# Splitting half of an expert's first w2 earlier, and longer filler runs of TensorE at the start, in an attention and two-MoE kernel

## The reference

```python
# attention in blocks of 64 tokens, 4 batches, 8 heads, 576 tokens, 64 features
scores = scale * np.matmul(q_c, k_c.transpose(0, 1, 2, 4, 3))
attn = softmax(scores); out = np.matmul(attn, v_c)
# x: 2304 tokens x 512 features
a = x @ w_a; b = x @ w_b          # 512 x 1536 each
x = a * b @ w_out                 # 1536 x 512
p = domain_probs / (domain_probs.sum(-1, keepdims=True) + 1e-09)
for e in range(4):                # w1[e]: 512 x 1024, w2[e]: 1024 x 512
    h = np.maximum(x @ w1[e], 0.0)
    out += p[:, e:e + 1] * (h @ w2[e])
```

## Time and profile before

| | us |
|---|---|
| median of 3 runs | 1179.96 |
| lowest, highest | 1179.81, 1180.49 |
| profiled execution, its own time | 1181.31 |
| span of its trace, first to last instruction | 1179.5 |
| TensorE busy in it | 1168.0 |
| VectorE, ScalarE busy | 858.8, 502.5 |
| mean granted TensorE clock | 0.998 of full speed |

### The profile page before, as it was taken

How to read it: one execution, slowest core, us unless ns; L and a number is a source line. 1 busy time by engine, 2 the same in 40 slices (tenths; PEclk the granted TensorE clock), 3 DMA queues, 4 the chain that set the end, 5 groups by cost and what they waited for, 6 DMA issues and landing times.

```text
span 1179.5 us, 18721 instructions
## 1 busy us (share of the span) xinstructions
PE 1168.0 (99%) x7577; PEld 1127.7 (96%) x7577; DVE 858.8 (73%) x1147; ACT 502.5 (43%) x869; POOL 0.7 (0%) x6
## 2 busy tenths in 40 slices
PE   8999999999999999999999999999999999999998
PEld 7999998889999889999999999999999999999997
DVE  5786789888788893367877777797346677777787
ACT  6555464445534542244444434444233533333332
POOL 0000000000000000000000000000000000000000
PEclk9999999999999999999999999999999999999999
DMA  7396785879877699938777777648894877676761
GB/s 270 118 348 239 284 321 222 327 301 348 339 300 271 260 412 362 331 131 324 307 262 251 279 279 274 241 166 285 254 356 170 340 264 263 251 266 250 262 252 55
DMA packets 73162, 319.54 MB, mean 271 GB/s; under 512 B 7340, under 2 KB 13812, under 8 KB 56692
## 3 DMA queue, kind: packets, MB, share of 16 engines
q1 hardware_dynamic: 72644, 317.56, 72.9%
q10 hardware_dynamic: 432, 0.79, 0.2%
HBM read 221.81 MB, written 96.51 MB: 270 GB/s over the span
## 4 chain that ended last, share of the span: by engine, by line
PE 91%; DVE 4%; DMA 2%; ACT 1%; issue 1%; SPq 0%; DVEq 0%; ACTq 0%
PE ps L672 30%; PE ps L674 29%; PE ps L673 29%; DMA kept_w<-w 1%; PE ps L701 1%; PE ps L682 1%; PE ps L690 1%; DMA kept_w<-lone 1%; DVE x L1654 0%; DVE h L1999 0%; PE ps L745 0%; PE ps L709 0%; ACT three L1099 0%; DVE hw L1654 0%; ACT hw L1099 0%
## 5 line engine op out<-in xcount | busy, mean ns | idle before, releaser
L672 PE MATMUL ps<-x,wab 128*128 128x384 f32 x504 | 169.3, 336 | 0.1
L674 PE MATMUL ps<-x,wab 128*128 128x384 f32 x504 | 168.4, 334 | 0.0
L673 PE MATMUL ps<-x,wab 128*128 128x384 f32 x504 | 168.4, 334 | 0.0
L1099 ACT ACTIVATE hw<-xraw 128x768 fp32r<-128x768 f32 x112 | 94.8, 847 | 163.3 <-DVE xraw L2137 80.7
L1099 ACT ACTIVATE ps<-ps 128x384 f32<-128x384 f32 (+1 forms) x184 | 91.3, 502 | 160.2 <-PE ps L674 157.1
L672 PE MATMUL ps<-hw,w2s 128*128 128x384 f32 x448 | 151.6, 338 | 0.0
L672 PE MATMUL ps<-x,w1s 128*128 128x384 f32 x448 | 151.6, 338 | 0.0
L674 PE MATMUL ps<-x,w1s 128*128 128x384 f32 x448 | 149.8, 334 | 0.0
L673 PE MATMUL ps<-x,w1s 128*128 128x384 f32 x448 | 149.7, 334 | 0.0
L674 PE MATMUL ps<-hw,w2s 128*128 128x384 f32 x448 | 149.7, 334 | 0.0
L673 PE MATMUL ps<-hw,w2s 128*128 128x384 f32 x448 | 149.7, 334 | 0.0
(11 more groups left out here) (198 smaller groups left out, 2252.9 us busy)
## 6 DMA issues: line engine op xcount, KB each, us to landing
wab<-kept_ab SPq DMA_DIRECT2D x70, 512.0 KB, 5.5
w1s<-kept_w SPq DMA_DIRECT2D x32, 1024.0 KB, 6.5
w2s<-kept_w SPq DMA_DIRECT2D x16, 2048.0 KB, 7.5
w1s<-kept_w SPq DMA_DIRECT2D x16, 1536.0 KB, 6.1
w2s<-kept_w SPq DMA_DIRECT2D x16, 1536.0 KB, 6.3
kept_ab<-wab SPq DMA_DIRECT2D x42, 512.0 KB, 5.3
raw<-in_w SPq DMA_DIRECT2D x16, 1024.0 KB, 10.2
kept_w<-w SPq DMA_DIRECT2D x16, 1024.0 KB, 12.3
```

Of the source, the lines that this page charges most:

```text
L672: pe.matmul(dst, stat(HI), mov(HI), start=first, stop=False, skip_group_check=True)
L673: pe.matmul(dst, stat(HI), mov(LO), start=False, stop=False, skip_group_check=True)
L674: return pe.matmul(dst, stat(LO), mov(HI), start=False, stop=last, skip_group_check=True)
L1099: return act.activation(dst, src, ACT.Copy)
```

## The change

Two things. The numbers of filler products between the pieces of the first three tiles go from 5, 7, 20, 9, 6, 5 to 6, 8, 36, 14, 10, 10. And the split of the first half of the first expert's w2 is made earlier: on ScalarE right behind the rounding of S3, ahead of phase 0's own work, and on VectorE between the rests of S2 and A12 in `finish_x2`. The second half stays where it was. Since this first half lies only over three of the six buffers of w_out, ScalarE waits for three stores instead of six.

```diff
@@ tensor @@
             score(0, 2)
-            keep_warm(5)
+            keep_warm(6)
             score(1, 4)
-            keep_warm(7)
+            keep_warm(8)
             score(2, 6)
-            keep_warm(20)
+            keep_warm(36)
             pe.wait_ge(ident_set, 1)
             turn_p(0, 0)
-            keep_warm(9)
+            keep_warm(14)
             turn_p(1, 1)
             attend(0, 2)
             attend(1, 4)
             turn_p(2, 0)
-            keep_warm(6)
+            keep_warm(10)
             attend(2, 6)
-            keep_warm(5)
+            keep_warm(10)
             make_unit(0, (0,))
@@ scalar, split_w2 @@
                     if w == 0:
-                        for i in range(FA - WRING, FA):
+                        for i in range(FA - WRING, FA - WRING + 3):
                             act.wait_ge(wo_moved[i % WRING], 16 * wo_stores(i))
@@ scalar, first_phase @@
                 if w == 0:
                     round_x2(2)
-                    split_w2(0, 0)
                     split_w2(0, 1)
@@ scalar, ahead of the phases @@
                     copy(x2[:, S3, HI], xr(2)).then_inc(x2_hi, 1)
+                    split_w2(0, 0)
```

## The result

The changed kernel took 1178.66 us in the median of 22 executions (1177.71 to 1179.53), the kernel before 1180.03 in 22 beside it (1179.28 to 1181.55). The ratio is 0.9986 with a 95% interval of 0.998 to 0.9992: 0.14% faster, which is clear of 1 and less than the 0.2% that I set as the bound of "same". The forecast was 1178.1 with a range of 1177.4 to 1179.6.

The account below looks back on a forecast made before the run. TensorE, busy 1168.0 of 1179.5 us, bounds the kernel, so only its idle time or a slower clock can be won. Fillers 1.2 plus w2's split 0.67 make 1.87 us off the 1179.96 median: 1178.1 us, range 1177.4 to 1179.6.

Parts of the forecast that it names:

- The fall of the clock: At the start, TensorE's granted clock of 0.50 from 13.6 to 17.0 us was predicted not to come with more fillers.
- the fillers' term: Holding the clock at the start was to bring unit 0 1.2 us earlier; bounds 0 and 1.7 us.
- The walk: Chain of the first three tiles retraced with durations at 2.4 GHz; unit 0 starts at 18.0 instead of 19.21 us.
- The stage of x2: Between unit 0 and phase 0 no gain of its own was forecast; earlier work just moves the end by as much.
- The direct cost of fillers: The 32 added fillers among the first three tiles end before what they precede and cost nothing directly.
- w2's split: In phase 0, VectorE's early rest of w2's half removes 1.14 us less 0.47 of delay: second part 0.67 us earlier.
- TensorE's cover enough for A12: In phase 0's first part, A12's rest comes later but 0.3 us of 0.8 us cover remain, so TensorE loses nothing.
- rival 1: At the start the clock falls all the same, only w2 counts: 1179.3 us; chance 0.28.
- 2: Clock falls earlier at the start and fillers at the low clock end late: 1179.9 us; chance 0.05.
- 3: w2 gives nothing in phase 0, since A12 or another operand is late on TensorE: 1178.8 us; chance 0.08.
- 4: w2's load lands late before A22's rounding on ScalarE, TensorE stands 6.1 us: 1184.9 us; chance 0.02.
- 5: More than forecast: both edits, at the start and in phase 0, reach their bounds, 2.54 us together: 1177.4 us; chance 0.07.

Follow-up runs that it names:

- load_late_before: Kernel before with w2's first load issued behind the stores of wo tile 11 and of its sums; 1179.77 us in one execution.
- split_only: Changed kernel with the old filler counts 5, 7, 20, 9, 6, 5, so only w2's first half split early; 1179.99 us, ratio 0.9995.
- short_run: Kernel before with 2 fillers in place of 20 ahead of the first turn; 1180.73 us, ratio 1.0005.
- fillers_only: Kernel before with all six filler counts of the change, w2 untouched; 1179.07 us, ratio 0.9989.
- first_run_only: Kernel before with 36 fillers in place of 20 ahead of the first turn, nothing else; 1179.41 us, ratio 0.999.
- later_runs_only: Kernel before with 14, 10 and 10 fillers in place of 9, 6 and 5, the run of 20 kept; 1179.62 us, ratio 0.9994.
- load_late: Changed kernel with w2's first load issued behind the stores of wo tile 11 and of its sums; 1178.82 us in one execution.
- long_run: Changed kernel with 60 fillers in place of 36 ahead of the first turn; 1180.54 us, ratio 1.0001.
- tail_back: Changed kernel with 60 fillers ahead of the first turn and the old 9, 6 and 5 behind the turns; 1179.55 us, ratio 0.9993.

## Why the prediction was right

**The fall of the clock.** I chose that it would not come, and it came in none of 22 executions. What I didn't see is that the kernel before has it in only 40 of 87. The one trace showed it, and I took it for the rule: the sum takes the price of a fall, read from an execution of 1181.31 us, off a median of 1179.96, whose three executions (1179.81 to 1180.49) by their times mostly had no fall. A term that is there in about half of the executions moves a median by something between nothing and its full size. So against the medians shown the fillers' term was worth less than the trace says in one batch and more in another: the medians of the kernel before run from 1180.03 to 1180.70.

**Its price.** The walk gave 18.0 for unit 0, that is 11.86 us behind the row maximum; it came at 12.04, and 1.03 us were won instead of 1.2. The missing 0.17 are small delays between an engine's release and its start that the walk left out. In whole executions the price is larger: those of the kernel before with and without the fall differ by 1.45 to 1.52 us. The traces of before and load_late_before, the same program up to unit 0, differ by 1.45 there too (19.21 against 17.76), but this holds 0.79 us by which the row maximum came later, and so the longer slow stretch at the start. How much of the 1.45 to 1.52 is that and how much the fall itself isn't shown.

**How much of the match is luck.** The forecast was a gain of 1.86 us, the medians give 1.37. The clocks of the 22 executions of the kernel before are not on record, but only four took over 1181 us, where those with a fall have their medians elsewhere. Without these four their median is 1179.96, and without the eight over 1180.45, the fastest at a clock of 0.997 in the other batches, 1179.86. By this estimate the fall moved this median by 0.1 to 0.2 us and w2 by 0.74, and some 0.5 us of the 1.37 are neither of my terms. A term that the forecast did not have stood in for most of the one that the median did not hold.

**The stage of x2, the part that I put at nothing.** I took it that behind the start and phase 0 all is only moved. But from unit 0 to phase 0 TensorE took 148.17, 148.39, 148.33 and 148.24 us in before, split_only, short_run and load_late_before, and 147.80 to 147.85 in the nine other traces that have no stop in unit 0. In this stage VectorE's sums of w_out wait for the store of the sums before: 3.13 to 3.38 us in those four traces, 1.47 to 2.26 in the ten others. The rows of before, load_late_before and fillers_only:

```profile
...
134.75 0.69 DVE L1869 TENSOR_TENSOR wo_three<-raw 128x512 f32<-128x512 f32 x1 [3.13 <-DMA kept_wo<-wo_lone]
```

```profile
...
133.41 0.69 DVE L1869 TENSOR_TENSOR wo_three<-raw 128x512 f32<-128x512 f32 x1 [3.26 <-DMA kept_wo<-wo_lone]
```

```profile
...
132.03 0.69 DVE L1869 TENSOR_TENSOR wo_three<-raw 128x512 f32<-128x512 f32 x1 [1.51 <-DMA kept_wo<-wo_lone]
```

It doesn't go with the fall, since load_late_before has the long wait with the clock at 1.00. It goes with the fillers: the four are all the kernels whose runs are nowhere longer than before, and first_run_only's 16 more, or the 14 more in all of later_runs_only, are enough for the short wait. The 0.3 to 0.6 us have the size of what the fillers give without a fall. How more fillers at 8 to 19 us shorten a wait at 132 us stays open.

**The direct cost of fillers, nothing.** Right: 36, 14, 10 and 10 end before what they stand ahead of, and unit 0 is as early in first_run_only as with all of them (12.04 us). That the later runs could be left out is what these traces say; their ten and eleven executions don't tell 1179.41 from 1179.07.

**w2's split.** 0.67 forecast, 0.74 measured between the same two matmuls, in the changed kernel and in split_only alike. The steps hold: A12's rest was to come 0.47 us late and came 0.42 late (it starts 2.02 us behind S2's, 1.60 before), S4's second idle time of 0.81 unchanged, TensorE's cover enough for A12. The remaining idle time in phase 0 was forecast at 0.1 to 0.2 us; TensorE was busy for 5.90 of the 6.00 us from 178 to 184.

**Does a gain early arrive at the end?** Yes, for both edits, to within what the last phase of the first stage adds of its own. TensorE's wait for L1999 there came out between 0.5 and 1.6 us in the traces in which that phase was left alone. Whether it differs between executions of one kernel or from kernel to kernel, one trace of each doesn't show; it blurs each comparison of two traces here.

**Rivals.** 1 and 2 (the clock falls all the same) fall with 0 of 22; the rule on transposes from the Trainium skill ("TensorE: Matmul & The Clock Gate", the part on PE-mode transpose) that stood beside rival 1 is neither shown nor contradicted by any run here, since the fillers alone could do it. 3 falls by the 0.74 us in the changed kernel and in split_only. 4 has its wait, and its 0.9 us of slack held in load_late; its price beyond that was not seen. 5 was not reached in the median (1178.66).

## What to carry to other kernels

A fall of TensorE's clock that one trace shows may be there in half of the executions: count it over the mean granted clock of many, and price it by executions of the same kernel with and without it. Filler products are free only up to the release that they wait beside, and their number can change waits far behind them, for the better (the stage of x2) or the worse (unit 0 in long_run), so compare executions without a fall as well before the gain is put down to the clock. To shorten the work ahead of a late operand, move a piece of it into idle time that the same engine has earlier, and count what is then behind it; moving it later instead gave the same wait back at the next operand, with interest.

## What the hardware showed unexpected

- The fall is a matter of chance with the idle stretch. By the mean granted clock it is there in 9 of 10 executions at about 2.8 to 3.0 us without a matmul, in 40 of 87 with the 20 fillers of the kernel before (1.5 to 2.0 us idle in the four traces with 20), in 1 of 10 in tail_back (whose 1180.16 us leaves it in doubt) and in none of the 87 other executions with 36 or 60 fillers ahead of the first turn. In each of the three traces that have it, it lasted 3.4 us at 0.50.
- The mean granted clock also counts a dip after the last matmuls. No matmul stands behind it to be slowed, but it can move the last digit of the mean: fillers_only has 0.999 without a fall at the start. A window of short_run over its last matmuls and the dip:

```profile
...
1172.00:1176.00 4.00, 1.60 (x10) 1.28 (x8) 4.00 (x6) 0.00 (x0) 0.00 (x0) 0.94 0.50 197
```

- TensorE stopped for 0.87 us within a run of twelve matmuls with nothing that it waited for, when its program had 24 fillers more ahead of them than the changed kernel (long_run), and not with 10 more (tail_back); one trace of each.
- VectorE's wait at 132 us for a store of w_out's sums was 3.13 to 3.38 us in the four traces whose filler runs are nowhere longer than before, and 1.47 to 2.26 us in the ten with more fillers.
